# The causal mask moves from a TensorE product into VectorE's maximum

## What is computed

```
scores = scale * np.matmul(q, k.transpose(0, 1, 3, 2))
causal = np.triu(np.ones((S, S), dtype=bool), k=1)
s_pos = np.maximum(s, 0.0)
cum = np.cumsum(s_pos, axis=-1)
bias = -(cum[:, :, :, None] - cum[:, :, None, :])
scores = np.where(causal, -1000000000.0, scores + np.minimum(bias, 0.0))
scores = scores - np.max(scores, axis=-1, keepdims=True)
attn = np.exp(scores)
attn = attn / (np.sum(attn, axis=-1, keepdims=True) + 1e-09)
return np.matmul(attn, v).astype(np.float32)
```

## Time and profile before

| | us |
|---|---|
| median of 3 runs | 554.97 (552.93 to 555.09) |
| the profiled execution | 555.02 |
| its span, first to last instruction | 553.2 |
| PE busy | 514.4 (93% of the span) |
| DVE busy | 392.2 (71%) |
| ACT busy | 328.7 (59%) |
| POOL busy | 257.7 (47%) |

### The profile page before, as it was taken

One profiled execution on the slowest core, in us unless ns is written; L12 is line 12 of the kernel. 1 busy time (PEld: TensorE's weight loads), 2 busy tenths in 40 slices (PEclk: granted clock), 3 DMA queues, 4 the chain that ended last, 5 costly groups with the idle time before them and its releaser, 6 DMA issues.

```text
span 553.2 us, 10378 instructions
## 1 busy us (share of the span) xinstructions
PE 514.4 (93%) x3472; PEld 453.2 (82%) x3472; DVE 392.2 (71%) x726; ACT 328.7 (59%) x844; POOL 257.7 (47%) x247
## 2 busy tenths in 40 slices
PE   1697998968999999999999999999999999999998
PEld 1475776747987999898888999898888999998997
DVE  7486699999666975888667957888567957665240
ACT  3777676765677655666667645775667456523322
POOL 5357453544667733634656635533657453104000
PEclk9999799977999999999999999999999999999999
DMA  6846356434533312345333332343343220200002
GB/s 187 229 128 151 71 140 169 118 83 108 153 83 84 86 42 68 78 130 131 87 88 87 88 87 54 88 110 106 80 104 84 73 67 12 87 11 2 1 2 85
DMA packets 46887, 50.34 MB, mean 91 GB/s; under 512 B 24881, under 2 KB 29137, under 8 KB 46834
## 3 DMA queue, kind: packets, MB, share of 16 engines
q1 hardware_dynamic: 46834, 49.68, 34.7%
HBM read 25.83 MB, written 4.95 MB: 56 GB/s over the span
## 4 chain that ended last, share of the span: by engine, by line
PE 50%; DVE 4%; issue 1%; ACT 0%; DVEq 0%; ACTq 0%
PE mix L1015 27%; PE attn_o L983 4%; PE score L1015 4%; PE turned L974 4%; PE attn_o L1015 4%; PE score L953 2%; DVE u_t L871 2%; PE score L954 1%; PE score L955 1%; PE score L962 1%; PE score L963 1%; DVE u_t L868 0%; DVE neg_max L825 0%; PE score L964 0%; PE attn_o L1005 0%
## 5 line engine op out<-in xcount | busy, mean ns | idle before, releaser
L697 ACT ACTIVATE prob<-score,neg_max 128x128 f32<-128x128 f32 (+4 forms) x159 | 89.7, 567 | 78.5 <-DVE neg_max L825 77.3
L825 DVE TENSOR_REDUCE neg_max<-score 128x1 f32<-128x128 f32 (+4 forms) x159 | 81.4, 533 | 52.9 <-PE score L964 26.6
L610 POOL TENSOR_TENSOR q<-raw,raw_hi 64x576 fp32r<-64x576 f32 x32 | 47.5, 1483 | 108.6 <-issue 91.9
L843 DVE TENSOR_TENSOR pt_lo<-turned,pt_hi 128x128 fp32r<-128x128 f32 (+4 forms) x160 | 72.7, 482 | 32.7 <-ACT pt_hi L706 32.6
L706 ACT ACTIVATE pt_hi<-turned 128x128 fp32r<-128x128 f32 (+4 forms) x160 | 62.6, 434 | 42.1 <-PE turned L974 41.7
L974 PE MATMUL turned<-ident,prob 128*128 128x128 f32 (+1 forms) x480 | 65.6, 268 | 17.3 <-DVE pt_lo L843 17.0
L871 DVE SCALAR_TENSOR_TENSOR u_t<-x_t,taps,u_t 128x576 f32<-128x576 f32 x64 | 77.4, 1210 | 1.8
L974 PEld LDWEIGHTS turned<-ident,prob 128*128 128x128 f32 (+1 forms) x480 | 52.5, 145 | 31.0 <-issue 19.7
L953 PE MATMUL score<-k,q 68*128 68x256 f32 (+2 forms) x128 | 53.8, 421 | 14.8 <-DMA k<-cum_dram 11.8
L983 PE MATMUL attn_o<-pt_hi,v_hl 128*128 128x256 f32 (+2 forms) x224 | 62.1, 297 | 0.0
L1015 PE MATMUL mix<-ws_hl,act_a 128*128 128x288 f32 (+1 forms) x405 | 59.9, 299 | 0.0
(11 more groups left out here) (149 smaller groups left out, 1020.8 us busy)
## 6 DMA issues: line engine op xcount, KB each, us to landing
q<-raw_hi SPq DMA_DIRECT2D x64, 144.0 KB
k<-raw_hi SPq DMA_DIRECT2D x64, 144.0 KB
raw<-in_q SPq DMA_DIRECT2D x32, 144.0 KB, 2.7
raw<-in_k SPq DMA_DIRECT2D x32, 144.0 KB, 2.9
r_bc<-r_dram SPq DMA_DIRECT2D x32, 144.0 KB, 3.3
out<-work SPq DMA_DIRECT2D x32, 144.0 KB, 1.8
v_raw<-in_v SPq DMA_DIRECT2D x32, 128.0 KB, 2.8
u_t<-in_moe_w_in SPq DMA_DIRECT2D x7, 256.0 KB, 5.1
```

The costliest lines, as they stand in the source:

```text
L610: pool.tensor_tensor(q2[p][0:D, :], raw[0:D, :], raw_hi[0:D, :].bitcast(F32), ALU.subtract).then_inc(lo_made, 1)
L697: act.activation(prob_view(i), score_view(g, i), ACT.Exp, bias=neg_max[p][0:rows[i], i:i + 1], accum_out=row_sum[p][0:rows[i], i:i + 1]).t ...
L825: dve.tensor_reduce(neg_max[g % 2][0:rows[i], i:i + 1], score_view(g, i), AX_X, ALU.max, negate=True).then_inc(max_done, 1)
L843: dve.tensor_tensor(pt_view(pt_lo, i), turned_view((g + i) % 2, i), pt_view(pt_hi, i).bitcast(F32), ALU.subtract).then_inc(pt_lo_done, 1)
```

## The change

VectorE adds the mask. Its operation `tensor_tensor_reduce` reads the scores from PSUM and a mask from SBUF, writes the negated sum to `prob`, and gives the minimum of each row, which is the negated maximum. ScalarE then takes the exponential of `prob` in place, with a scale of -1. The score banks come free with the maximum (`max_done`) and no longer with the exponential (`exp_done`). Since VectorE now writes `prob`, it waits for the transposes of the head before (`turned_done`), as ScalarE did. `mask_b` grows to 640 columns, zeros ahead of the triangle, so that each tile reads a slice of its own width; `pt_hi` and `pt_lo` shrink from 2112 to 1856 columns by another layout of their blocks, and `turn` writes its blocks in the reverse order for tiles 2 to 4.

```diff
 def pt_view(t, i):
     if i < 2:
-        part = t[:, 0:PT_A].rearrange("p (j c) -> p j c", c=QA)
+        part = t[:, PT_B:PT_LEN].rearrange("p (j c) -> p j c", c=QA)
         return part[:, 0:i + 1, P * i:P * (i + 1)]
-    part = t[:, PT_A:PT_LEN].rearrange("p (j c) -> p j c", c=QB)
-    return part[:, 0:i + 1, P * (i - 2):P * (i - 2) + rows[i]]
+    at = late_at(i) + P * (i - 2)
+    return t[:, at:at + (i + 1) * QB].rearrange("p (j c) -> p j c", c=QB)[:, :, 0:rows[i]]
...
-    pool.affine_select(out=mask_b[:], in_=mask_b[:], compare_op=ALU.is_ge, fill=MASKED, base=0,
-                       pattern=[[-1, P]], channel_multiplier=1).then_inc(pool_sets, 1)
+    pool.affine_select(out=mask_b[:, FULL * P:], in_=mask_b[:, FULL * P:], compare_op=ALU.is_ge, fill=MASKED,
+                       base=0, pattern=[[-1, P]], channel_multiplier=1).then_inc(pool_sets, 1)
     pool.wait_ge(pool_sets, 5)
-    pool.tensor_copy(ident_b[:], ident[:]).then_inc(pool_sets, 1)
-    pool.wait_ge(pool_sets, 6)
...
 def exp(g, i):
-    wait(act, turned_done, NT * (g - 1) + i + 1)
-    act.activation(prob_view(i), score_view(g, i), ACT.Exp, bias=neg_max[p][0:rows[i], i:i + 1],
+    act.activation(prob_view(i), prob_view(i), ACT.Exp, bias=neg_max[p][0:rows[i], i:i + 1], scale=-1.0,
                    accum_out=row_sum[p][0:rows[i], i:i + 1]).then_inc(exp_done, 1)
...
 def scores(g, i):                      # VectorE
     dve.wait_ge(scores_done, NT * g + i + 1)
-    dve.tensor_reduce(neg_max[g % 2][0:rows[i], i:i + 1], score_view(g, i), AX_X, ALU.max,
-                      negate=True).then_inc(max_done, 1)
+    wait(dve, turned_done, NT * (g - 1) + i + 1)
+    if g == 0 and i == 0:
+        dve.wait_ge(pool_sets, 5)
+    at = FULL * P + P - width[i] if i < FULL else 0
+    dve.tensor_tensor_reduce(prob_view(i), score_view(g, i), mask_b[0:rows[i], at:at + width[i]], -1.0, -LEAST,
+                             ALU.add, ALU.min, neg_max[g % 2][0:rows[i], i:i + 1]).then_inc(max_done, 1)
...
 def comb_mm(n, kk):
-        pe.wait_ge(exp_done, NT)
+        pe.wait_ge(max_done, NT)
...
 def scores(g, i):                      # TensorE
     if i == NT - 1:
-        wait(pe, exp_done, NT * g + (0 if roomy(g) else 4))
+        wait(pe, max_done, NT * g + (0 if roomy(g) else 4))
     else:
-        wait(pe, exp_done, NT * g + last_users[i])
+        wait(pe, max_done, NT * g + last_users[i])
...
-        pe.matmul(score[:, base:base + n], q2[p][:, qs], k2[p][:, 0:n], start=False, stop=False)
-        ins = pe.matmul(score[:, base + P * i:base + P * (i + 1)], ident_b[:, :], mask_b[:, :],
-                        start=False, stop=True)
+        ins = pe.matmul(score[:, base:base + n], q2[p][:, qs], k2[p][:, 0:n], start=False, stop=True)
...
-            pe.matmul(o, q2[p][:, qs], k2[p][:, ks], start=False, stop=(half == 0))
-        ins = pe.matmul(last[:, S - LAST:S], ident_b[0:LAST, 0:LAST],
-                        mask_b[0:LAST, 0:LAST], start=False, stop=True)
+            ins = pe.matmul(o, q2[p][:, qs], k2[p][:, ks], start=False, stop=True)
...
 def turn(g, i):                        # TensorE
-        ins = pe.transpose(turned[:, (g + i) % 2, j * rows[i]:(j + 1) * rows[i]],
+        to = (i - j if i >= 2 else j) * rows[i]
+        ins = pe.transpose(turned[:, (g + i) % 2, to:to + rows[i]],
```

More of the change, by code:

```diff
@@ L28 @@
 MASKED = -1.0e9
+LEAST = -3.0e38
 SUM_EPS = 1.0e-9
@@ L132, in build @@
     O_OFF = BANK - QA
-    PT_A = 2 * QA
-    PT_LEN = PT_A + NT * QB
+    PT_B = FULL * QB + LAST
+    PT_LEN = PT_B + 2 * QA
     UNITS = [("val", m, side) for side in range(2) for m in range(NC)] + [("v", j, 0) for j in range(NT)] + \
@@ L205, in build @@
         ident = sb("ident", [P, P], F32)
-        ident_b = sb("ident_b", [P, P], BF16)
-        mask_b = sb("mask_b", [P, P], BF16)
+        mask_b = sb("mask_b", [P, FULL * P + P], BF16)
         r_dram = nc.dram_tensor("r_dram", [NH, NT * P], F32, kind="Internal").ap()
@@ L282, in chan, with late_at @@
             return t[:, hl, c * S:(c + 1) * S]
+        def late_at(j):
+            return (FULL - j) * QB - 2 * P
         def pt_view(t, i):
             if i < 2:
-                part = t[:, 0:PT_A].rearrange("p (j c) -> p j c", c=QA)
+                part = t[:, PT_B:PT_LEN].rearrange("p (j c) -> p j c", c=QA)
                 return part[:, 0:i + 1, P * i:P * (i + 1)]
-            part = t[:, PT_A:PT_LEN].rearrange("p (j c) -> p j c", c=QB)
-            return part[:, 0:i + 1, P * (i - 2):P * (i - 2) + rows[i]]
+            at = late_at(i) + P * (i - 2)
+            return t[:, at:at + (i + 1) * QB].rearrange("p (j c) -> p j c", c=QB)[:, :, 0:rows[i]]
         def turned_view(bank, i):
@@ L808, in later_setup @@
                 for t in (pt_hi, pt_lo):
-                    dve.memset(words(t[:, QA:QA + P]), 0.0).then_inc(zeroed, 1)
-                    dve.memset(words(t[:, PT_A + 3 * QB + D:PT_A + 3 * QB + P]), 0.0).then_inc(zeroed, 1)
+                    dve.memset(words(t[:, PT_B + QA:PT_B + QA + P]), 0.0).then_inc(zeroed, 1)
+                    dve.memset(words(t[:, late_at(3) + D:late_at(3) + P]), 0.0).then_inc(zeroed, 1)
                 dve.memset(words(ws_hl[LAST:LAST + 2, 1, FULL * S:NT * S]), 0.0).then_inc(zeroed, 1)
@@ L919, in setup @@
             def setup():
-                pe.wait_ge(pool_sets, 6)
+                pe.wait_ge(pool_sets, 5)
             def comb_mm(n, kk):
@@ L980, in pv_part @@
                     lo, hi = (0, QA) if first else [(QA, S), (QA, S), (QA, S), (QA + D, S), (FULL * P, S)][j]
-                    at = QA * j + lo if first else PT_A + QB * j + lo - QA
+                    at = PT_B + QA * j + lo if first else late_at(j) + lo - QA
                     for t in (pt_hi, pt_lo):
```

## The result

The changed kernel takes 535.49 us (median of 4 runs, 534.49 to 539.67) against 554.64 before. The ratio, taken over all runs and not from the two medians, is 0.9674, with a 95% interval of 0.9619 to 0.9730. The forecast was 542.5 us, in a range of 535.5 to 551, so this time stands at the range's very edge. Timed twice more beside the experiments, the same changed kernel stood at 0.9704 (0.9668 to 0.9739) and at 0.9735 (0.9701 to 0.9770). On the 555.0 us of the prediction the three ratios are 536.9, 538.6 and 540.3 us. So the gain is 15 to 18 us where the sum had 12.6, and the first measurement shows the largest gain of the three.

What follows compares the result with a forecast made beforehand. VectorE was taken to bound 76 to 134 us, TensorE 134 to 467 us. Savings of 17.4 less 3.4 and 1.4, with 0 early, took 12.6 off 555.0: 542.4 us, stated as 542.5, range 535.5 to 551.

Steps and rivals of the forecast that it cites:

- Part 1: TensorE, 134 to 467 us: removing 88 mask products at 0.12 us and 22 at 0.31 saves 17.4 us.
- Part 2: At seven head changes VectorE's queue sets the end, so TensorE waits instead of gaining: 3.4 us of 17.4 lost.
- the seven places: Head changes behind 134 us where convolution steps stand between two `pt_lo` steps and VectorE has nearly no gap.
- the three places like head 13: Of the seven, those where TensorE just avoids waiting for `pt_lo`: slack of 0.15 us each, taken off the loss.
- the two like head 23: Of the seven, places where TensorE already waits before a transpose (0.99 us in head 23): 0.55 us lost each.
- Part 3: VectorE's new operation: body at 0, each row-minimum read 0.10 us; 14 reads at the seven places cost 1.4 us.
- Part 4: Before 134 us: 22 reads cost 2.2 us from 76 us on, offset by small gains; sum 0.
- the 2.2 us that were given back: Early offsets to the reads: 1.2 us for VectorE idle time and sooner scores, 1.0 for masks from 24 to 76 us.
- Part 5: Edits priced at nothing: VectorE's new wait, the layout, and ScalarE's exponential from SBUF, 22 ns x 160 hidden by idle time.
- The waits spread (A): Rival, chance 0.20: the order fits the old pace, so waits appear throughout the heads; 549 us, or 554 with no change.
- The scan's rate (B): Rival, chance 0.10: VectorE's new operation runs as slowly per column as the scan; slower, 557 us.
- More gain (C): Rival, chance 0.12: the read is free or hidden and the seven places give way; 535.4 us.

Runs made afterwards that it cites:

- the kernel with both masks: Changed kernel with the mask products put back on TensorE, so the mask is added twice; 553.36 us, ratio 0.9992 to the kernel before.
- ten real steps of 0.08 us: Changed kernel with a small reciprocal, result unused, behind each of the 160 new VectorE operations; 539.81 us, ratio 0.9773 to the kernel before.
- no mask at all: Kernel before with its mask products left out and nothing in their place; 538.73 and 538.78 us, ratios 0.9741 and 0.9717.

## Why the prediction was right, and where its size was off

**Part 1, the price of the mask products: right.** 16.6 us were foreseen for the 84 and 21 products of the late part; TensorE's busy time fell by 16.6. Each kind alone gave 0.12 and 0.30 us, against 0.12 and 0.31.

**Part 2, what the seven places keep: right in the mechanism and the sum, not in the split.** 3.4 us were foreseen; TensorE's idle time in the late part grew by 3.2, and all its new waits are at the seven places. But the waits before transposes grew by less than foreseen: by 0.29 us in the three places like head 13 (0.55 - 0.15 = 0.40 foreseen) and by 0.39 in the two like head 23 (0.55 foreseen); the 0.7 us each, reads included, that was to show the prediction right was not met. In the other two, heads 17 and 25, TensorE waits not before a transpose but before a `mix` product, for VectorE's `u_t`, and there the waits grew from 1.3 us to 3.1 in all, where 1.1 more was foreseen. That the sum came out is in part luck. With convolution steps moved away from these places, and nothing else changed, 5.4 us came back, of which the kernel before had 3.2 to gain as well.

**Part 3, the row minimum: mis-sized, and this is the term that failed.** "I take 0.10 us" was put for each read. It was foreseen as a separate instruction held as long as a small operation, and it is a separate instruction, but it starts together with the next operation. From start to start the new operation is 8 ns longer than the old maximum at 256 columns (349 against 341), and the kernel with both masks has the ratio 0.9992. What the prediction concluded from the passage that it cites, that the 0 is out, was wrong: a second instruction need not have a price. The body at 0 was right, 685 against 680 ns. My bound from below, 0, was the better value; the reciprocal of the earlier trace rows was a wrong neighbour, because it is a whole operation of its own. The term was also put in the wrong place: ten real steps of 0.08 us at five of the seven places did not lengthen TensorE's waits, so even a read with a price would not have cost 14 times that price there.

**Part 4, the early part: off by the same term, and blind to the clock.** The 2.2 us for 22 reads from 76 to 134 us were not paid. The prediction named a fall of the granted clock behind a longer wait as what would spoil the sum, and put nothing down for it. It came about in the early part: without its mask products TensorE waits longer for VectorE (15.2 us before transposes from 24 to 132 us, 10.8 before in the earlier trace rows), and from 80 to 112 us its clock is 0.89. It is 0.89 there in all three profiles of the changed kernel and in both with no mask at all, whose VectorE work is the old one, and 1.00 with both masks (80 to 114 us), so it comes from leaving out the products and not from the new operation. What it costs is not shown, since VectorE is the bound there for most of the time; an estimate is the 1.4 us by which VectorE is idle for longer in that stretch (2.8 against 1.4). What is left of the term is the 2.2 us that were given back, which the runs can neither confirm nor refute: one kernel's early part varies by 3 us. By the ratios, 15 to 18 us less the late part's 13 leave 2 to 5.

**The sum.** With the read at 0 the prediction gave 538.8 us; the three measurements of the changed kernel stand at 536.9, 538.6 and 540.3 when their ratios are put on its 555.0. The first measurement was 535.5, the range's lower edge; the 542.5 lies above all three. Of the 7 us between 542.5 and 535.5, some 3.7 are the mis-sized term, and the rest is not more than the scatter between measurements. The direction and the mechanism carried the forecast; that the first time fell just on the range's edge and not beyond it is luck.

**Part 5: right.** The exponential of 512 columns takes 716 ns from SBUF, 30 more than from PSUM (22 foreseen), which ScalarE's idle time hides; no wait of TensorE names it.

**The rivals.** The waits spread (A): not so; all the new waits of the late part are at the places named. The scan's rate (B): not so, 685 ns at 512 columns. More gain (C): its time was met in the first measurement, and of its mechanism only the free read; the seven places did not give way, they had to be given room.

## What to carry to other kernels

Price a small product on a full TensorE by the starts around it, the second one behind it included: these cost 0.12 and 0.30 us, with 0.04 of the first in its own place. Before counting on the gain, look for the places where another engine's queue is full and TensorE arrives just in time; a fixed order has to be loosened there for the rest of the gain (here 2.2 us of the change's own, and 3.2 that were to be had before it). Taking work off an engine where it is not the bound makes it wait longer there, and here its clock fell with that (from 1.00 to 0.89 between 80 and 112 us). And when whole times scatter by more than the step in question, cut the traces at an event behind the scatter.

## What the runs showed that I had not expected

VectorE's read of an accumulator, 82 ns, starts at the same time as the next operation and costs next to nothing, while a reciprocal of 128 x 1 in the same spot takes its 0.08 us from start to start. Writing 512 columns to SBUF beside the reduction, and reading a second input for it, added 5 ns to the 680 of the maximum alone. The 64 x 64 mask product, the smallest of all, was the dearest one: 0.30 us for each, more than twice the 128 x 128 one's 0.12.
